# A different order for GpSimd in each attention unit, and the loads for its value sums issued first

## What is computed

```python
    q_d = q.reshape(B, H, Sd, factor, D).mean(axis=3)   # factor = 4, k_d and v_d alike
    out_d = sm_attn(q_d, k_d, v_d)
    out_up = np.repeat(out_d, factor, axis=2)
    mask = np.abs(pos[:, None] - pos[None, :]) < factor
    scores = np.where(mask, scale * np.matmul(q, k.transpose(0, 1, 3, 2)), -1000000000.0)
    ...
    out_local = np.matmul(attn, v)
    return (out_up + out_local).astype(np.float32)
```

## Time and profile before

| | us |
|---|---|
| median of 3 runs | 949.58 |
| lowest and highest | 945.84, 951.64 |
| the profiled execution | 949.2 |
| its span, first to last instruction | 947.1 |
| mean granted TensorE clock | 0.971 |
| TensorE matmul busy | 901.8 (95%) |
| GpSimd busy | 300.5 (32%) |

### The profile page before, as it was taken

The page is one execution under the profiler, slowest core; times in us unless marked ns, Lnnn a source line. Parts: engine busy times, 40 slices in busy tenths (PEclk is TensorE's granted clock), DMA queues, the critical chain, the costliest instruction groups (busy, mean ns, idle before and its releaser), DMA issues.

```text
span 947.1 us, 15642 instructions
## 1 busy us (share of the span) xinstructions
PE 901.8 (95%) x6056; PEld 844.4 (89%) x6056; DVE 577.1 (61%) x901; ACT 387.3 (41%) x750; POOL 300.5 (32%) x251
## 2 busy tenths in 40 slices
PE   7877787999999999999998999999999999999997
PEld 5766577989999999999998999999999999999996
DVE  8777745666876566866668555556544456544445
ACT  4765645443533234433334544444322234222221
POOL 5978677674102000111015555741200001000000
PEclk8898969999999999999999999999999999999999
DMA  9677628667746464645421567679775555575411
GB/s 259 170 217 218 168 77 306 222 237 261 275 153 227 147 228 151 221 158 211 165 92 45 217 262 279 274 292 365 282 285 208 217 214 214 212 279 201 199 45 67
DMA packets 46089, 197.01 MB, mean 208 GB/s; under 512 B 3936, under 2 KB 15552, under 8 KB 33216
## 3 DMA queue, kind: packets, MB, share of 16 engines
q1 hardware_dynamic: 41984, 166.66, 48.9%
q0 software_dynamic: 4032, 29.36, 8.3%
HBM read 139.90 MB, written 56.10 MB: 207 GB/s over the span
## 4 chain that ended last, share of the span: by engine, by line
PE 79%; POOL 9%; DVE 3%; DMA 3%; issue 3%; ACT 2%; SPq 0%; POOLq 0%; DVEq 0%; ACTq 0%
PE banks L787 43%; PE banks L855 18%; PE banks L971 16%; DMA v_four<-in_v_dram 2%; POOL v_four L554 1%; POOL win L595 1%; POOL prob L561 1%; POOL mid L601 1%; POOL v_down L558 1%; ACT win L1035 1%; PE banks L765 1%; DMA qk<-in_k_dram 1%; POOL prob_d L561 1%; DVE x_op L1297 1%; PE banks L742 0%
## 5 line engine op out<-in xcount | busy, mean ns | idle before, releaser
L787 PE MATMUL banks<-x_op,pair 128*128 128x384 f32 x1512 | 278.5, 336 | 1.7 <-DVE cg_sum L1457 1.7
L787 PEld LDWEIGHTS banks<-x_op,pair 128*128 128x128 f32 x1512 | 266.7, 189 | 9.7 <-DVE cg_sum L1457 2.1
L855 PE MATMUL banks<-g_parts,mid 128*128 128x384 f32 x1152 | 228.4, 337 | 7.3 <-DVE x_all L1377 5.3
L855 PEld LDWEIGHTS banks<-g_parts,mid 128*128 128x128 f32 x1152 | 203.0, 189 | 10.2 <-DVE x_all L1377 7.3
L787 PE MATMUL banks<-x_op,win 128*128 128x384 f32 x1008 | 206.7, 342 | 4.3 <-ACT c_sum L1071 4.3
L787 PEld LDWEIGHTS banks<-x_op,win 128*128 128x128 f32 x1008 | 182.3, 193 | 5.5 <-ACT c_sum L1071 3.8
L971 PE MATMUL banks<-wout,p_parts 128*128 128x512 f32 x648 | 163.6, 393 | 1.7 <-issue 1.7
L1377 DVE TENSOR_TENSOR x_all<-banks,x_all 128x384 f32<-128x384 f32 x168 | 93.0, 555 | 83.3 <-PE banks L855 82.9
L971 PEld LDWEIGHTS banks<-wout,p_parts 128*128 128x128 f32 x648 | 120.3, 188 | 22.6 <-issue 2.1
L1482 DVE TENSOR_TENSOR x_all<-banks,x_all 128x512 f32<-128x512 f32 x90 | 62.1, 690 | 113.4 <-PE banks L971 113.4
L617 POOL DMA_DIRECT2D wout<-kept_out x12 | 6.4, 537 | 211.4 <-PE banks L971 211.4
(11 more groups left out here) (93 smaller groups left out, 1008.8 us busy)
## 6 DMA issues: line engine op xcount, KB each, us to landing
pair<-kept_pair SPq DMA_DIRECT2D x24, 1792.0 KB, 10.8
win<-kept_in SPq DMA_DIRECT2D x16, 1792.0 KB, 7.4
kept_pair<-pair SPq DMA_DIRECT2D x12, 1792.0 KB, 11.8
mid<-kept_mid POOLq DMA_DIRECT2D x16, 1024.0 KB, 5.1
kept_in<-win SPq DMA_DIRECT2D x7, 1792.0 KB, 6.8
wout<-kept_out POOLq DMA_DIRECT2D x12, 1024.0 KB, 11.7
kept_mid<-mid SPq DMA_DIRECT2D x7, 1024.0 KB, 7.0
kept_out<-wout SPq DMA_DIRECT2D x6, 1024.0 KB, 14.6
```

What stands on the lines that cost most here:

```text
L787: mm = pe.matmul(bk[:, 0:T], weights[:, w, p - 1, kk, :], x_op[:, p - 1, x, kk, :], start=(first and kk == 0 and a == 0), stop=(last and k ...
L855: mm = pe.matmul(bk[:, 0:T], w[:, wp, f, m * P:(m + 1) * P], g[:, gp, 2 * f + t, :], start=(f == 0 and a == 0), stop=(f == 1 and a == 2))
```

## The change

In GpSimd's iteration `denominators` and `normalise` of a unit come ahead of its `value_sums`. In SP's loop `load_v_four(u + 1)` is issued ahead of `load_v(u)`. Waits and buffers stay as they are.

```diff
@@ SP @@
             for u in range(UNITS):
                 if u + 3 < UNITS:
                     load_qk(u + 3)
-                load_v(u)
                 if u + 1 < UNITS:
                     load_v_four(u + 1)
+                load_v(u)
                 if u == 0:
                     load_raw(0)
@@ GpSimd @@
             for t in range(UNITS + 1):
                 if t > 0:
-                    value_sums(t - 1)
                     denominators(t - 1)
                     normalise(t - 1)
+                    value_sums(t - 1)
                 if t == 2:
                     weight_sums(0)
```

## The result

The changed kernel takes 987.14 us (median of 4, 985.28 to 988.72), against 948.71 for the kernel before in the same comparison. The ratio is 1.0404, with a 95% interval of 1.0363 to 1.0446: 4% slower, 38 us. The profiled execution took 988.72, 39.5 more than the one shown before.

The account below looks back on a forecast made before the run. The prediction took v_four transfers and value sums to bound units 6 to 9, GpSimd idling 14.2 us. Unit 14's value products 15.7 us later plus 4.1 for the clock, 19.8 on 949.2, gave 969 us; range 952 to 984.

Parts of the forecast that it names:

- V(0): Value sums of unit 0 on GpSimd, now behind that unit's normalising; forecast to end at 18.1 us.
- B: Rival: v_win loads on the path, but overlapping other transfers, x near 3.0 us; 952 us; chance 0.13.
- C: Rival: v_win lands in under 2.7 us and no longer binds, only normalising's freedom counts; 948 us; chance 0.04.
- A: The prediction's own case: v_win loads on the path with x of 4.2 to 5.4 us; 960 to 984 us; chance 0.78.
- D: Rival: low clock in nearly every loop, x at 5.4 us or above, stores competing; over 984 us; chance 0.05.
- x: Time from a unit's value sums ending to its value products starting, for v_win behind v_four; 4.7 us, counted eight times.
- The clock: TensorE's attention work partly at the lower clock, 2.1 us more per loop, seven loops; 4.1 us, bounds 0 and 14.7.
- GpSimd's other work: Weight-block work, x sums and x_low beside the attention units; extras forecast to delay unit 14's value products by 5.5 us.
- a(11): Start of the value products of unit 11 on TensorE; forecast at 107.4 us.
- N(13): Normalising of unit 13 on GpSimd, with two x_low instructions ahead of its row sum; forecast at 118.9 us.
- LV(u): The three v_win loads of unit u on SP's queue; forecast not to be issued before that unit's value sums end.
- L4(u): The v_four load of unit u on SP's queue; with the value sums, forecast as a loop of 5.8 us in either order.

## Why the prediction was right or wrong

The direction and the mechanism came out. V(0) ended at 18.38 us (forecast 18.1). v_win is the releaser of the value products in every even unit, GpSimd's wait for v_four nearly went, the loop has the links that were named, the MLP stages took up nothing, and the way from value products to normalising is 5.67 us where the clock is full (5.8). B and C were not it. A had the mechanism, but its sizes are those of D, "low clock in nearly every loop and x at 5.4 or above", which had a chance of 0.05. D's reason for the long x, stores that compete, was not tested.

The size was wrong by nearly a factor of two: 19.8 us forecast, 38 measured, outside the range. Against the forecast start of unit 14's value products, 134.0 + 4.1 = 138.1 us, the trace has 157.93, 19.8 more, in three terms.

- **The clock, the step that failed most.** "A mean of 0.86 is the lower level, half speed, for about 28% of the time (0.14 of 0.5); 0.28 x 7 x 2.1 is 4.1 us, an estimate." Measured is 9.02 - 5.67 = 3.35 us in each of seven pairs, 23.5 us. The share was taken from a kernel without this wait, where the change itself creates a wait of 2.6 to 6 us ahead of each loop's TensorE part: it is 7 of 7 and not 0.28. With that share alone put right the term would be 7 x 2.1, the 14.7 us that the prediction named as its upper bound. The other 8.8 us come from a second omission: the 2.1 us scaled only the value products and local scores. The sum had let VectorE's maxima cover the turning (L742) and the averaged scores (L731). With the turning at half clock the averaged scores are late, and VectorE's last maximum waits for them: in unit 6 it starts at 90.13 us, 0.52 us after VectorE was free. Against what the forecast had for this way, that is 7 x 9.02 = 63.1 us in place of 7 x 5.8 + 4.1 = 44.7, or 18.4 us more.
- **x.** 4.7 was taken from a range of 4.2 to 5.4. Over the even units it measured 5.16 to 6.66, 5.57 in the mean, above the range. Eight times 0.87 is 7.0 us. q and k in the place of v_win set the range too low: k's landing, 5.4, was nearer than the value between them. The fit in the Trainium skill, "DMA: Bandwidth & Descriptors", "Anatomy of one DMA — SWDGE (gpsimd) path", is stated for DMAs that GpSimd issues. Taken for SP's loads it had given an estimate of 3.4, further from the measured 5.57 still.
- **GpSimd's other work.** 5.5 us were put on the even chain for the x sums and x_low. None of it is there: the loop got so slow that idle time hides it. The x sums end at 107.0 us, and unit 10's normalising starts at 110.09, after VectorE. The two x_low instructions lengthen the odd chain (10.65 us from a(11) to N(13)), but V(13) ends at 143.37, 4.4 us ahead of N(14).

18.4 + 7.0 - 5.5 is 19.9, the missing 19.8 but for rounding.

Beside these three, what the prediction treated as the present bound, the v_four loop of the earlier trace rows, was only nearly one: with a second buffer the kernel before gains nothing. It also read the place of v_win in the kernel before too freely. "Before, its own wait was only for the value products two units back, and LV(u) was issued some two units ahead of its use": in SP's old order LV(u) stands behind L4(u), which waits for V(u-1), and LV(6) went out 9.15 us ahead, 1.3 units of 7.1. So v_win hung on the value sums already, in a longer loop, and that either order alone is nearly harmless was not seen.

## What to carry to other kernels

Ahead of moving a load behind a waiting instruction of its queue, follow what that wait hangs on after the other moves too: one order alone cost 0.9% here, the other nothing that could be measured, and the pair 4%, because only the pair shortens the loop through the wait to two units. The time of one turn must be divided by the number of rounds that it spans. Where a change puts a wait of some microseconds ahead of TensorE's work in every round, price that work at the lower clock in every round, and redo the maximum over engines with it, since what another engine covered at full clock may come out on the path. If the order must stay, a second buffer that moves the wait a unit back is the cure, and it took the whole loss away here.

## What the runs showed of the hardware

The clock did not fall at one fixed place. In unit 6 of the changed kernel it fell at the end of the wait, at about 82.3 us, and in unit 4 earlier, at about 62 us of a wait that ended at 63.36; in the run with six matmuls of filler it was 1.00 through the rest of 2.25 us and at the first value products (79.14), and 0.50 from 80.0 us on, while TensorE was busy. A small transfer was not quick behind others: the last 35 KB of v_win, issued 1.2 us after the 288 KB of v_four and behind 245 KB more, were in use 5.1 to 6.6 us after the issue of v_four.
